# A fused attention and expert kernel: positions ahead of scaling, and transposes of zeros in the opening's idle stretches of the matmul engine

## The chip, the cores and the metric

The kernel runs on one core of a Trainium2 chip. The metric is the device time of one execution in microseconds (us); for the kernel before it is the median of three runs. The profile is of one execution, and its times count from the start of that execution's span. Engines are named TensorE (PE, with PEld for its weight loads), VectorE (DVE), ScalarE (ACT), GpSimd (POOL) and SyncE (SP).

## The reference

Three stages follow one another. The first is a linear attention with a complex decay for each position and dimension, the second a choice of one expert out of eight per token, the third a feed forward layer.

```python
mag = np.sqrt(a_re * a_re + a_im * a_im)
scale = np.minimum(mag, 0.999) / (mag + 1e-06)
for t in range(S):                      # B, H, S, D = 4, 8, 768, 48
    S_re = ar * S_re - ai * S_im + k[t] v[t]^T
    S_im = ar * S_im + ai * S_re
    y[t] = q[t] @ S_re
x = y as (3072, 384)
e = argmax(x @ w_gate);  x = gate_w * sigmoid(x @ w_output_gate) * relu(x @ w1[e]) @ w2[e]
out = max(0.01 * (x @ w_in), x @ w_in) @ w_out
```

## The kernel before

The kernel does not run the recurrence step by step. It takes chunks of 128 positions, 24 in all (`NCH`), where chunk `n` belongs to batch `n % 4`. Within a chunk the logarithm of the decay and its angle are summed over positions by a matmul with the triangle `tri`. Queries are multiplied by the exponential of the summed logarithm (`fall`), keys by its inverse (`rise`); that is `scale` (L883). Both are rotated by the summed angle (`rotate`, L896). Then the chunk is an ordinary masked attention plus a state carried from chunk to chunk.

The coefficients `a_in` pass through a long chain of elementwise work, in units of one chunk (the first two) or two chunks: squares and logarithms on ScalarE (L636 to L646), the signed numerator, the cap and the negative logarithm on VectorE (`numerator` L841, `cap` L848, `decay_log` L855), a difference and a product on GpSimd (`cosine_log` L483, `sine_eps` L492), the tangent of half the angle on VectorE (L862), the arctangent on ScalarE (L656) and the turn on VectorE (L870). GpSimd's `sine_eps(u)` waits, from unit 3 on, for the count `s_qe` of scaled queries, that is for `scale(n + 1)` of the chunk in which it stands.

TensorE sums the logarithms (`sum_logs`, L1096) and the turns (`sum_turns`, L1106); each sum is one call, which the profile shows as two matmul records. It transposes rotated queries and keys (`transposes`, L1136 and L1138), which ScalarE and VectorE copy from the banks (`query` L696, `first_key` L703 into `k_t`, `second_key` L919), computes scores (L1119), outputs (L1164, L1169), the update of the state (L1178) and the logits (L1189, L1191). Each chunk is done in two halves of four heads.

Each engine works through an order written out by hand, and semaphores tie the orders together. The opening prepares units 0 to 2 and chunk 0 ahead of the loop; TensorE's part of it is seven calls (L1203 to L1209), each of which waits for its own input. In the loop VectorE's order for chunk `n` is: add the state's update, `mask`, `second_key`, the cap and the negative logarithm (even chunks), turns (odd chunks), `scale(n + 1)`, in some chunks `positions`, then `rotate(n + 1)` and the second mask.

`positions` (L946) belongs to the routing of tokens. For each group of four chunks TensorE computes ranks (`ranks`, L1200 and L1201), in chunks 6, 10, 14 and 18 ahead of the second scores, and VectorE makes positions of them with three instructions: a product, a sum, and a conversion to integers (L951). TensorE's update in that chunk waits for them (L1174), since the ranks lie in the same bank, and GpSimd needs them for the scatter of rows one chunk later. For the fifth group `positions` stands at L1035, ahead of the scaling, in chunk 21.

`zeros` is a tile of 128 x 386 which SyncE stores past the end of the sorted rows (L446) and, later, behind each expert's region. It is written in GpSimd's order behind the first six elementwise passes and the triangle `stri`.

Behind the attention come a table of blocks, the experts' two layers (L2060, L2070, L2082) with weights that GpSimd splits into two parts (L1843, L1845) into a buffer that TensorE has released, and the feed forward layer (L2102, L2115).

Of the kernel before, what the change touches and what calls it, by code (L numbers as in the profile page):

```python
# [17 lines left out]
C = P  # L18
# [164 lines left out]
def attention(nc, ctx, sem, sb, in_a, in_qkv, wg_pairs, bank, ident, tri, stri, ones, wgp_sb, flag, stage, wm, moe_w, xs,  # L183
# [3 lines left out]
    sc_bank, y_bank, u_bank, cum_bank = bank[4], bank[5], bank[6], bank[7]  # L187
# [65 lines left out]
    s_lnu = sem("log_of_square")  # L253
# [3 lines left out]
    s_nl = sem("neglog_ready")  # L257
    s_flip = sem("left_half_plane")
    s_num = sem("signed_imaginary_part")
# [58 lines left out]
    def fallen(n):  # L318

        if n == 0:  # L320
            return [2, 3, 4, 5]
        return [n + 4, n + 5] if n % 2 == 0 and n + 4 < NCH else []
# [142 lines left out]
    def scan_gpsimd(pool):  # L465
# [3 lines left out]
        pool.memset(log_eps[:, :], math.log(MAG_EPS)).then_inc(s_bias, 1)  # L469
        pool.memset(rounder[:, :], ROUND).then_inc(s_bias, 1)  # L470
        pool.memset(least_run[:, :], 3.0e38).then_inc(s_bias, 1)
        pool.memset(tri[:, :], 1.0).then_inc(s_const, 1)
        pool.memset(ident[:, :], 0.0).then_inc(s_const, 1)
        pool.wait_ge(s_const, 2)
# [91 lines left out]
        for u in range(3):  # L566
# [3 lines left out]
        pool.wait_ge(s_const, 6)  # L570
        pool.affine_select(out=stri[:, :], in_=stri[:, :], compare_op=ALU.is_gt, fill=0.0, base=0,
                           pattern=[[1, P]], channel_multiplier=-1).then_inc(s_const, 1)
        pool.memset(zeros[:, :], 0.0).then_inc(s_idle, 1)
        pool.iota(order[:, :], [[-1, E]], base=E, channel_multiplier=0,
                  allow_small_or_imprecise_dtypes=True).then_inc(s_k, 1)
        pool.iota(region[:, :], [[REG, E]], base=0, channel_multiplier=0,
# [242 lines left out]
    def scan_vector(dve):  # L819
# [63 lines left out]
        def scale(m):  # L883
            if not real(m):
                return
            dve.wait_ge(s_qkv[m % RING], 16 * (m // RING + 1))
            dve.wait_ge(s_rise, m + 1)
            need(dve, s_kr, 2 * m)
            dve.tensor_tensor(kh_bank[:, 0:W], qkv_in[m % RING][:, 1, :], rise[m % FALLS][:, :],
                              ALU.mult).then_inc(s_ke, 1)  # L890
            dve.wait_ge(s_fall, m + 1)
            need(dve, s_qr, 2 * m)
            dve.tensor_tensor(qh_bank[:, 0:W], qkv_in[m % RING][:, 0, :], fall[m % FALLS][:, :],
                              ALU.mult).then_inc(s_qe, 1)
# [51 lines left out]
        def positions(g):  # L946
            ranked = by_token(ranked_parts, g, E)
            dve.wait_ge(s_rank, g + 1)
            step(dve.tensor_tensor(ranked, ranks_at(g), of_group(pick, g), ALU.mult))
            step(dve.tensor_reduce(of_group(posf, g), ranked, AX_X, ALU.add))  # L950
            dve.tensor_copy(of_group(pos, g), of_group(posf, g)).then_inc(s_pos, 1)  # L951
# [74 lines left out]
        for n in range(NCH + 1):  # L1026
            add_update(n - 1)
            if n % 2 == 1:
                out_copy(n - 1)
            mask(n, 0)  # L1030
            second_key(n)
            if n % B == 3 and B < n < NCH - 1:
                gate_rows(n // B - 1)
            if n in (NCH - 3, NCH - 1):
                positions(GLAST - 2 + (n - NCH + 3) // 2)  # L1035
            if n == NCH - 2:
                gate_rows(GLAST - 2)
            if n == NCH:
                gate_rows(GLAST - 1)
                pick_experts(GLAST)  # L1040
                region_ends()
                positions(GLAST)
                gate_rows(GLAST)
            if chain_exp(n) is not None:
                cap(chain_exp(n))
                decay_log(chain_exp(n))
            if chain_angle(n) is not None:
                turns(chain_angle(n))
            scale(n + 1)
            if n % B == 2 and B < n < NCH - 2:  # L1050
                positions(n // B - 1)
            if n % 2 == 0:
                rotate(n + 1)
                mask(n, 1)
                u = chain_exp(n)
                if u is not None:
                    half_tangent(u)
                for m in summed(n):
                    phases(m)
                if n % B == 0 and 0 < n < NCH:  # L1060
                    pick_experts(n // B - 1)
                if n == NCH - 2:
                    pick_experts(GLAST - 1)
            else:
                rotate(n + 1)
                mask(n, 1)
                u = chain_log(n)
                if u is not None:
                    left_half(u)
                    sum_squares(u)  # L1070
                for m in summed(n):
                    phases(m)
                if u is not None:
                    numerator(u)
            if n in (NCH - 3, NCH - 2):
                first_trailing(n - NCH + 3)
            if n == NCH - 3:
                dve.wait_ge(s_u, len(units))
                dve.tensor_scalar(strong[:, :], least_run[:, (len(units) - 1) % 2:(len(units) - 1) % 2 + 1], WEAKEST,
                                  None, ALU.is_gt).then_inc(s_strong, 1)  # L1080
            if n == NCH - 2:

                dve.wait_ge(s_weak, 1)
                dve.tensor_scalar(flag[:, :], cum_bank[0:1, 0:1], float(P), None, ALU.is_lt).then_inc(s_flag, 1)

    def scan_tensor(pe):
        pe.wait_ge(s_const, 4)

        def sum_logs(m):
            pe.wait_ge(s_nl, unit_of(m) + 1)  # L1090
            if m == 3:
                pe.wait_ge(s_ph, 3)
            if m > 3:
                pe.wait_ge(s_kt[1], m - 3 - m % 2)
                pe.wait_ge(s_qt, 2 * (m - 3 - m % 2))
            pe.matmul(cum_of(m, 0)[:, 0:W], tri[:, :], neglog[pair(unit_of(m))][:, ccols(m)], start=True,  # L1096
                      stop=True).then_inc(s_cl, 1)

        def sum_turns(m):
            pe.wait_ge(s_turn, unit_of(m) + 1)  # L1100
            need(pe, s_carried, m - B + 1)
            if m in (2, 3):
                pe.wait_ge(s_rise, 1 if m == 2 else 4)
            if m > 3:
                pe.wait_ge(s_ph, m)
            pe.matmul(cum_of(m, 1)[:, 0:W], tri[:, :], turn[pair(unit_of(m))][:, ccols(m)], start=True,  # L1106
                      stop=True).then_inc(s_ct, 1)
# [15 lines left out]
        def transposes(n, h):  # L1123
            if not real(n):
                return
            pe.wait_ge(s_qr, 2 * (n + 1))
            pe.wait_ge(s_kr, 2 * (n + 1))
            need(pe, s_qt, 2 * n + h)
            if n == 0:
                pe.wait_ge(s_ph, 2)  # L1130
            need(pe, s_kt[1 - h], n + h)
            if h == 0 and n % 2 == 1 and n + 3 < NCH:
                pe.wait_ge(s_rise, n + 5)
            for a in range(HH):
                head = h * HH + a
                pe.transpose(qt_bank[0:2 * D, a * C:(a + 1) * C],  # L1136
                             qr[n % 2][:, head, :, :].rearrange("p c d -> p (c d)"), ident[:, :])
                last = pe.transpose(kt_bank[0:2 * D, a * C:(a + 1) * C],  # L1138
                                    kr[n % 2][:, head, :, :].rearrange("p c d -> p (c d)"), ident[:, :])
            last.then_inc(s_tqk, 1)  # L1140
# [54 lines left out]
        def ranks(g):  # L1195
# [4 lines left out]
            pe.matmul(ranks_at(g), stri[:, :], of_group(pick, g), start=True, stop=False)  # L1200
            pe.matmul(ranks_at(g), ones[:, :], acc[:, n * E:(n + size) * E], start=False, stop=True).then_inc(s_rank, 1)  # L1201

        sum_logs(0)  # L1203
        sum_logs(1)
        sum_turns(0)
        sum_turns(1)
        sum_logs(2)
        sum_turns(2)
        transposes(0, 0)  # L1209

        for n in range(NCH + 1):
            scores(n, 0)
            if n == 0:
                sum_logs(3)
            transposes(n, 1)
            logits(n - 1)
            if n % B == 2 and B < n < NCH - 2:
                pe.wait_ge(s_su, min(n, LAST))
                ranks(n // B - 1)
            if n in (NCH - 3, NCH - 1):  # L1220
                pe.wait_ge(s_su, LAST)
                ranks(GLAST - 2 + (n - NCH + 3) // 2)
            scores(n, 1)
            for m in fallen(n):
                if m > 3:
                    sum_logs(m)
            outputs(n, 0)
            if n % 2 == 0:
                for m in summed(n):
                    sum_turns(m)  # L1230
            transposes(n + 1, 0)
            if n % 2 == 1:
                for m in summed(n):
                    sum_turns(m)
            if n == NCH - 2:
                pe.wait_ge(s_strong, 1)
                pe.wait_ge(s_const, 7)
                pe.wait_ge(s_ph, NCH)
                pe.matmul(cum_bank[:, 0:1], ones[:, :], strong[:, :], start=True, stop=True).then_inc(s_weak, 1)
            outputs(n, 1)  # L1240
# [971 lines left out]
```

## Time and profile before

| | us |
|---|---|
| median of three runs | 1013.23 |
| lowest and highest | 1013.14, 1015.47 |
| the profiled execution, its own time | 1014.68 |
| its span, first to last instruction | 1012.7 |
| TensorE busy (matmuls) | 941.1, 93% |
| GpSimd, ScalarE, VectorE busy | 505.5, 453.9, 415.9 |

The span has four stretches. The opening lasts until the loop over chunks is under way, some 45 us. The attention runs to about 293 us. Some 20 us of table, tails and first block follow, in which TensorE has almost nothing to do, and then the experts and, from 593 us, the feed forward layer, with TensorE busy throughout. A busy TensorE in this profile is not TensorE at its peak: the same matmuls take twice as long at the lower of its two clocks.

A row of a timeline gives the start, the duration (of several instructions in a row, if they are merged: x4), the engine, the line, the operation and the tiles, and in brackets how long the engine had idled and what ended that. A row of the chain gives start, length and the piece of work that the end of the program waited for. Clock columns give the granted clock as a share of the full 2.4 GHz.

### The profile page before, as it was taken

How to read it: one execution, taken by the hardware profiler on the slowest of the kernel's cores; microseconds unless marked ns; L12 is line 12 of the kernel's file. 1: busy time of each engine (PE TensorE's matmuls, PEld its weight loads, DVE VectorE, ACT ScalarE, POOL GpSimd, SP SyncE). 2: the span in 40 equal slices, each digit the busy share in tenths (PEclk: the TensorE clock that was granted, in tenths of full speed). 3: DMA queues.
4: the chain of work that ended last, by engine and by line, in shares of the span. 5: the costliest groups of instructions: out<-in, count | busy, mean ns of one | idle time of the engine just before them, and what ended most of it. 6: DMA issues, size and time to landing. Idle time of an engine off the chain costs nothing.

```text
span 1012.7 us, 17328 instructions
## 1 busy us (share of the span) xinstructions
PE 941.1 (93%) x5836; PEld 832.5 (82%) x5837; DVE 415.9 (41%) x742; ACT 453.9 (45%) x772; POOL 505.5 (50%) x429
## 2 busy tenths in 40 slices
PE   1899999999838999999999999999999999999995
PEld 0677778887736999998998989999999999999995
DVE  6698998998844233233232322212112121121110
ACT  7899888897612232232222333333333333333322
POOL 4134565565556568568839943342342433433433
PEclk9999999999978999999999999999999999999998
DMA  4542463430252343343534520010010100000000
GB/s 149 166 134 80 124 214 103 112 110 17 100 171 96 106 163 107 103 163 104 155 114 163 186 57 17 16 39 16 9 39 17 39 16 17 32 1 1 32 1 32
DMA packets 47190, 84.04 MB, mean 83 GB/s; under 512 B 23812, under 2 KB 36376, under 8 KB 44568
## 3 DMA queue, kind: packets, MB, share of 16 engines
q1 hardware_dynamic: 40984, 48.59, 16.0%
q0 software_dynamic: 6144, 34.65, 9.7%
q8 instruction: 37, 0.61, 0.3%
q14 instruction: 25, 0.20, 0.1%
HBM read 65.80 MB, written 17.38 MB: 82 GB/s over the span
## 4 chain that ended last, share of the span: by engine, by line
PE 72%; ACT 10%; issue 6%; DVE 6%; POOL 4%; SPq 1%; DMA 1%; POOLq 0%; DVEq 0%; ACTq 0%
PE bank L2102 20%; PE bank L2115 19%; PE bank L2060 11%; PE bank L2082 10%; POOL wm L1845 3%; PE bank L2070 2%; PE bank L1136 1%; PE bank L1119 1%; PE bank L1138 1%; POOL wm L1843 1%; PE bank L1096 1%; DVE neglog L848 1%; PE bank L1178 1%; PE bank L2036 1%; PE bank L1106 1%
## 5 line engine op out<-in xcount | busy, mean ns | idle before, releaser
L1871 POOL TENSOR_TENSOR act_r<-act_f,act_r 128x512 fp32r<-128x512 f32 x96 | 124.4, 1296 | 260.5 <-ACT act_r L1930 257.8
L2115 PE MATMUL bank<-w_out_r,act_r 128*128 128x384 f32 x1152 | 217.7, 337 | 0.3 <-POOL act_r L1871 0.3
L2102 PE MATMUL bank<-x,w_in_r 128*128 128x512 f32 x864 | 216.7, 395 | 0.0
L2115 PEld LDWEIGHTS bank<-w_out_r,act_r 128*128 128x128 f32 x1152 | 204.8, 188 | 8.8 <-POOL act_r L1871 0.6
L1991 DVE TENSOR_TENSOR act_f<-bank,small 128x512 f32<-128x512 f32 x96 | 66.4, 692 | 292.7 <-ACT small L1927 275.2
L2102 PEld LDWEIGHTS bank<-x,w_in_r 128*128 128x128 f32 x864 | 159.6, 188 | 29.4
L1927 ACT ACTIVATE small<-bank 128x512 f32<-128x512 f32 x96 | 57.4, 598 | 191.5 <-PE bank L2102 191.4
L2060 PE MATMUL bank<-wm,x_tr 128*128 (+1 forms) x522 | 129.1, 401 | 4.0 <-POOL wm L1845 1.7
L2082 PE MATMUL bank<-wm,h_tr 128*128 (+1 forms) x696 | 128.6, 339 | 0.7 <-DVE h_tr L1975 0.7
L2082 PEld LDWEIGHTS bank<-wm,h_tr 128*128 128x128 f32 x696 | 120.1, 188 | 1.0 <-issue 1.0
L2060 PEld LDWEIGHTS bank<-wm,x_tr 128*128 128x128 f32 x522 | 97.6, 191 | 24.8 <-issue 5.0
L1845 POOL TENSOR_TENSOR wm<-stage,wm 128x3072 fp32r<-128x3072 f32 x14 | 95.3, 6808 | 1.2
L1930 ACT ACTIVATE act_r<-act_f 128x512 fp32r<-128x512 f32 x96 | 60.7, 632 | 72.8 <-DVE act_f L1991 72.8
L1907 ACT ACTIVATE h_tr<-bank 128x512 fp32r<-128x512 f32 x58 | 31.6, 596 | 120.5 <-PE bank L2070 120.5
L1843 POOL TENSOR_SCALAR wm<-stage 128x3072 fp32r<-128x3072 f32 x14 | 38.9, 2780 | 71.3 <-PE bank L2082 56.3
L1902 ACT ACTIVATE h<-bank 128x512 f32<-128x512 f32 x58 | 31.5, 596 | 71.4 <-PE bank L2060 71.4
L1119 PE MATMUL bank<-q_t,k_t 96*128 96x128 f32 x384 | 56.2, 291 | 4.5 <-ACT q_t L696 2.7
L1981 DVE COPY y_b<-bank 128x384 f32<-128x384 f32 x29 | 16.2, 558 | 95.1 <-PE bank L2082 80.4
L1136 PE MATMUL bank<-ident,qr 128*96 128x128 f32 x192 | 46.8, 282 | 7.3 <-DVE qr L911 7.3
L1119 PEld LDWEIGHTS bank<-q_t,k_t 96*128 96x128 f32 x384 | 48.3, 197 | 6.1 <-ACT q_t L696 4.2
L1966 DVE CAST x_tr<-bank 128x384 fp32r<-128x384 f32 x30 | 16.7, 558 | 80.5 <-PE bank L2036 80.5
L1975 DVE TENSOR_TENSOR h_tr<-bank,h_tr 128x512 fp32r<-128x512 f32 x58 | 37.4, 686 | 21.3 <-ACT h_tr L1907 21.0
(193 smaller groups left out, 1378.1 us busy)
## 6 DMA issues: line engine op xcount, KB each, us to landing
stage<-moe_w POOLq DMA_DIRECT2D x12, 1536.0 KB, 7.0
qkv_in<-in_qkv SPq DMA_DIRECT2D x24, 576.0 KB, 5.5
a_in<-in_a SPq DMA_DIRECT2D x11, 768.0 KB, 5.3
stage<-moe_w SPq DMA_DIRECT2D x4, 1536.0 KB
x_b<-x_sorted SPq DMA_DIRECT2D x30, 193.0 KB
y_sorted<-y_b SPq DMA_DIRECT2D x29, 192.0 KB
xg<-y_sorted SPq DMA_DIRECT2D x24, 192.0 KB, 2.4
stage<-w_out POOLq DMA_DIRECT2D x2, 1536.0 KB, 7.1
```

The source lines that it names most:

```text
L1119: last = pe.matmul(sc_bank[:, a * C:(a + 1) * C], k_t[h][:, a * C:(a + 1) * C], q_t[h][:, a * C:(a + 1) * C], start=True, stop=True)
L1136: pe.transpose(qt_bank[0:2 * D, a * C:(a + 1) * C], qr[n % 2][:, head, :, :].rearrange("p c d -> p (c d)"), ident[:, :])
L1843: pool.tensor_scalar(lead, half, 1.0, 0.0, ALU.mult, ALU.add).then_inc(s_ws, 1)
L1845: pool.tensor_tensor(trail, half, lead.bitcast(F32), ALU.subtract).then_inc(s_wh, 1)
L1871: pool.tensor_tensor(a[:, 1, :], act_f[f % 2][:, :], a[:, 0, :].bitcast(F32), ALU.subtract).then_inc(s_gl, 1)
L1927: act.activation(small[f % 2][:, :], h_bank[f % 2][:, :], ACT.Copy, scale=0.01).then_inc(s_c, 1)
L1930: act.activation(act_r[f % 4][:, 0, :], act_f[f % 2][:, :], ACT.Copy).then_inc(s_gh, 1)
L1991: dve.tensor_tensor(act_f[f % 2][:, :], h_bank[f % 2][:, :], small[f % 2][:, :], ALU.max).then_inc(s_g, 1)
L2060: last = pe.matmul(hid_bank[j][:, :], x_tr[:, xp, t * P:(t + 1) * P], wmf[:, part_of(base, wp * WE + t * F1 + j * 512, 512)], start=(t == ...
L2082: last = pe.matmul(ye_bank[:, 0:W], h_tr[:, hp, t * P:(t + 1) * P], wmf[:, part_of(base, wp * WE + t * W, W)], start=(t == 0 and n == 0), ...
L2102: last = pe.matmul(h_bank[f % 2][:, :], w_in_r[:, wp, t * F2 + f * P:t * F2 + (f + 1) * P], window_part(w, xp)[:, t, :], start=(t == 0 and ...
L2115: last = pe.matmul(o_bank[j][:, 0:W], a[:, ap, j * P:(j + 1) * P], w_out_r[:, wp, f * W:(f + 1) * W], start=(f == 0 and n == 0), stop=(f = ...
```

## The change

`positions` goes ahead of `scale(n + 1)` in VectorE's order, in chunks 6, 10, 14 and 18. TensorE gets eleven groups of transposes, 144 in all, each behind a wait for a count that another engine raises. They read the tile of zeros and write into the output bank, which holds zeros until chunk 0's outputs. The memset of the zeros moves to the start of GpSimd's order, since the transposes read the tile from the first group on. In the loop only chunk 0 has groups of transposes.

```diff
@@ scan_gpsimd
         pool.memset(least_run[:, :], 3.0e38).then_inc(s_bias, 1)
+        pool.memset(zeros[:, :], 0.0).then_inc(s_idle, 1)
         pool.memset(tri[:, :], 1.0).then_inc(s_const, 1)
...
-        pool.memset(zeros[:, :], 0.0).then_inc(s_idle, 1)
@@ scan_vector
                 turns(chain_angle(n))
-            scale(n + 1)
             if n % B == 2 and B < n < NCH - 2:
                 positions(n // B - 1)
+            scale(n + 1)
@@ scan_tensor
+        def keep_warm(count, event, value):
+            pe.wait_ge(event, value)
+            for i in range(count):
+                pe.transpose(y_bank[:, i % 4 * C:(i % 4 + 1) * C], zeros[:, 0:C], ident[:, :])
+        pe.wait_ge(s_clear, 1)
+        pe.wait_ge(s_idle, 1)
+        keep_warm(28, s_num, 1)
         sum_logs(0)
         sum_logs(1)
+        keep_warm(20, s_nl, 2)
+        keep_warm(16, s_ratio, 1)
+        keep_warm(8, s_ratio, 2)
+        keep_warm(14, s_atan, 2)
         sum_turns(0)
         sum_turns(1)
         sum_logs(2)
+        keep_warm(8, s_rnd, 1)
+        keep_warm(10, s_rnd, 2)
         sum_turns(2)
+        keep_warm(10, s_turn, 3)
         transposes(0, 0)
+        keep_warm(16, s_qr, 2)
         for n in range(NCH + 1):
             scores(n, 0)
             if n == 0:
                 sum_logs(3)
             transposes(n, 1)
+            if n == 0:
+                keep_warm(8, s_qt, 1)
             logits(n - 1)
...
             scores(n, 1)
+            if n == 0:
+                keep_warm(6, s_lnu, 4)
             for m in fallen(n):
```

The counts are `s_num` of numerators, `s_nl` of negative logarithms, `s_ratio` of tangents, `s_atan` of arctangents, `s_rnd` of rounded angle sums, `s_turn` of turns, `s_qr` of rotated halves of queries, `s_qt` of copies into `q_t`, and `s_lnu` of logarithms.

## Rows read from the trace of the kernel before

**Rows 1.** The page: the chain by engine, and the weights' first pass on GpSimd.
```profile
PE 72%; ACT 10%; issue 6%; DVE 6%; POOL 4%; SPq 1%; DMA 1%; POOLq 0%; DVEq 0%; ACTq 0%
...
L1843 POOL TENSOR_SCALAR wm<-stage 128x3072 fp32r<-128x3072 f32 x14 | 38.9, 2780 | 71.3 <-PE bank L2082 56.3
```

**Rows 2.** The chain that ended last, 22 to 60 us: start, length, piece.
```profile
23.49 2.94 PE bank L1106 x4
...
30.87 0.45 PE bank L1136
...
32.85 0.60 ACT q_t L696
...
34.03 2.05 PE bank L1119 x8
36.07 1.28 PE bank L1096 x2
...
41.93 2.00 PE bank L1096 x4
```

**Rows 3.** The timeline of the opening, rows of four engines.
```profile
7.20 1.02 DVE L841 SCALAR_TENSOR_TENSOR a_in<-flip,a_in 128x384 f32<-128x384 f32 x2
...
14.24 2.90 PE L1096 MATMUL bank<-neglog,tri 128*128 128x384 f32 x4 [14.24 <-DVE neglog L855]
...
20.65 0.94 ACT L656 ACTIVATE main<-main 128x384 f32<-128x384 f32 x2
...
21.20 0.41 POOL L573 MEMSET zeros<- 128x386 f32 x1
...
37.15 1.81 POOL L483 TENSOR_TENSOR main<-main,log_sq 128x768 f32<-128x768 f32 x1 [14.57 <-ACT main L642]
...
39.10 0.59 ACT L696 ACTIVATE q_t<-bank 96x512 f32<-96x512 f32 x1 [1.27 <-PE bank L1138]
...
40.28 0.96 DVE L855 SCALAR_TENSOR_TENSOR neglog<-neglog,eps_mag 128x768 f32<-128x768 f32 x1
```

**Rows 4.** Busy time, clock and DMA by stretch, around the attention's end.
```profile
289.00:290.00 1.00, 0.00 (x0) 0.00 (x0) 0.58 (x4) 0.40 (x3) 0.71 (x3) 0.50 0.28 105
...
313.00:314.00 1.00, 1.00 (x6) 0.84 (x5) 0.00 (x0) 0.00 (x0) 0.95 (x1) 1.00 0.00 0
```

**Rows 5.** Transposes of 128x128: timeline at the low clock, chain at full clock.
```profile
305.54 0.90 PE L2036 MATMUL bank<-ident,x_b 128*128 128x128 f32 x3 [13.10 <-ACT x_b L1897]
...
345.14 0.87 PE bank L2070 x8
```

**Rows 6.** The timeline of chunk 6, and of chunk 21's conversion.
```profile
101.33 1.82 POOL L483 TENSOR_TENSOR main<-main,log_sq 128x768 f32<-128x768 f32 x1
...
102.29 1.27 DVE L848 TENSOR_SCALAR neglog<-log_sq 128x768 f32<-128x768 f32 x1
...
104.61 1.56 PE L1096 MATMUL bank<-neglog,tri 128*128 128x384 f32 x4 [0.33 <-DVE neglog L855]
...
105.67 1.81 POOL L492 TENSOR_TENSOR a_in<-a_in,eps_mag 128x768 f32<-128x768 f32 x1 [2.53 <-DVE bank L893]
...
105.86 1.66 DVE L951 CAST pos<-posf 128x4 int32<-128x4 f32 x1
...
107.57 0.88 PE L1178 MATMUL bank<-qkv_in,kr 128*96 128x48 f32 x8 [0.38 <-DVE pos L951]
...
111.03 0.58 ACT L703 ACTIVATE k_t<-bank 96x512 f32<-96x512 f32 x1
...
264.56 0.17 DVE L951 CAST pos<-posf 128x4 int32<-128x4 f32 x1
```

**Rows 7.** The conversion's line over the whole span.
```profile
L951 DVE CAST pos<-posf x7: 169/1659/1668, 105.9 to 293.0; 128x4 int32<-128x4 f32 x5, 128x2 int32<-128x2 f32 x2
```

**Rows 8.** The chain of chunk 8.
```profile
126.95 1.56 PE bank L1096 x4
...
132.45 0.58 ACT k_t L703
```

## The prediction

> **What bounds the kernel now.** I read the page first. The chain that ended last is 72% TensorE, and where it passes through GpSimd, which splits the experts' weights, that work waited for TensorE to release a buffer [rows 1]. So behind the attention nothing runs on a clock of its own, and a shift made early should arrive at the end. The change works before 44 us and at four points of the attention; the question is what the chain goes through there.
>
> The chain of the opening [rows 2] goes through TensorE in five pieces between 23.49 and 43.93 us, with short pieces of ScalarE and VectorE between them, and TensorE's pieces are slow. Four records of the turn sums take 2.94 us; four of the same shape take 1.56 in chunk 8 [rows 8]: a factor of 1.88. The clock column of the opening is no help (it shows 1.00 before the first matmul has run); where it does report, it falls from 1.00 to 0.50, the 1.2 GHz level, when the attention's matmuls stop, and is back at 1.00, 2.4 GHz, at 313 us, after work that began at 305.54, with one pause [rows 4, 5]. The opening's durations are those of the low level. The last piece holds the return: four records in 2.00 us are two at 0.64, as at 36.07, and two at 0.36, so the clock rose near 43.2. Before that TensorE idled until 14.24, and again from 17.14, where the log sums end, to 23.49, 6.35 us [rows 2, 3].
>
> Chunk 6 shows the other part [rows 6, 7]. VectorE's conversion of positions, 128x4 elements, takes 1.66 us. Of seven the median is 1659 ns and the shortest 169, so four are long. The long one starts at 105.86, behind the start of GpSimd's product (105.67), and ends at 107.52 with it (107.48). That product waits for `scale(n + 1)`, and `positions` stands right behind `scale(n + 1)`: they meet each time. It reaches the chain: from the start of the log sums to the copy into `k_t` chunk 6 takes 111.03 - 104.61 = 6.42 us, chunk 8, which has no positions, 132.45 - 126.95 = 5.50 [rows 8].
>
> **Positions ahead of scaling.** Nothing is added; three VectorE instructions pass two others, in chunks 6, 10, 14 and 18. They wait for the ranks, which stand in TensorE's queue ahead of a set of scores of about 1 us that is done 0.33 before 104.61; VectorE arrives at 104.5. No wait is added. GpSimd is idle for the 2.53 us before its product, so the conversion finds it idle. From the conversion to the next instruction is 1.57 us today (to 107.43, where the product releases it) and 0.11 behind a short one (chunk 21, where it stands ahead of the scaling) [rows 6]. VectorE gains 1.46. The scaling comes about 0.56 later: the conversion's 0.11 and two small steps of some 0.22. Three things hang on it: GpSimd's product (from 106.2 to 108.0, and the pass that needs it comes near 108.4), ScalarE's fall of chunk `n + 5` (behind log sums that end at 106.17, the scaling ends at 106.0), and the rotation, done near 107.9. Each has room. TensorE gains less than VectorE: its stall of 0.38 before the update goes, and then it is itself what is late, with update and turn sums in front of the next transposes. That is chunk 8's pattern, so I take the difference of the two chunks, 0.92. Bounds: 0, if the conversion stays long against something else, and 1.46, all that VectorE gains. 4 x 0.92 = 3.7 us, between 0 and 5.8.
>
> **The memset moved.** 0.41 us on GpSimd [rows 3], now ahead of `tri` and `ident`, which are ready some 2 us into the span and first wanted at 7.7; the bias columns, for which ScalarE waits, are written before it. Where it stood, GpSimd idles for 14.57 us afterwards. Nothing either way.
>
> **144 transposes.** A 128x128 transpose costs 0.21 at the low clock (three take 0.90 with the tail of the last, about 0.47) and 0.109 at the full one (eight take 0.87) [rows 5]. The first 28 follow the first numerator, at 7.7 us, and take 6.0 at the low clock, to 13.7, in front of the log sums at 14.24. From 7.7 on TensorE is all but never idle. The clock came back 7.5 us after the start of such work at 305.54, so I expect it by 15 to 17. Then come 20 (2.2 us), 16 (1.7), 8 (0.9), and 14 (1.5) behind the second arctangent at 21.6 [rows 3], done by 23.2: the turn sums lose nothing. From there, in order.
>
> Turn sums: 2.94 becomes 1.56, 1.4 gained, and phases, turns and the rotation follow, ended by 29.45. TensorE meanwhile does a log sum (25.05 to 25.8), 8 and 10 transposes (27.7), a turn sum (28.5) and 10 more: 29.6, so 0.15 is lost. The eight transposes of chunk 0, 1.96 today, take 1.0 and end at 30.6 instead of 32.83: 2.2 earlier.
>
> ScalarE's two copies would let the scores start at 31.8, but 16 transposes last until 32.35: 1.7 earlier. Scores, a log sum and eight transposes, 5.04 today (34.03 to 39.07), take 2.65 and end at 35.0: 4.1 earlier.
>
> Now ScalarE is late. It ends its exponential 1.27 before the copy at 39.10 [rows 3], at 37.83, and follows its own `k_t` copy, so 35.6: the copy starts at 35.65, 3.45 earlier. VectorE caps the logarithm meanwhile, and should meet GpSimd's difference (1.81 long [rows 3], from 34.95), as in chunk 6, where the cap takes 1.27 beside it [rows 6]; it ends at 36.8, and the pass behind it (0.96) has the negative logarithm ready at 37.8 instead of 41.24. Scores end near 37.45, six transposes at 38.1, and the log sums run to 39.7 instead of 43.93: 4.2 earlier. From here the work is the same, at the full clock.
>
> So 4.2 us. Upper bound: all slow pieces at the full clock and nothing lost, (2.94 + 1.96 + 5.04 + 2.05) x 0.47 + 0.44 = 6.1. Lower: 1.4, if the turn sums gain and groups that overrun eat the rest. Loads are no limit: each idle stretch in these rows ends with an engine.
>
> **Sum.** 4.2 + 3.7 = 7.9 us off the profiled execution's 1014.68 (span 1012.7) is 1006.8. That execution is 1.45 above the median of the three, 1013.23, so the median comes to 1005.3.
>
> **A rule against it.** All that fills the gaps is transposes, and no stretch of the trace has transposes alone, so it cannot show that they raise the clock. From 34.03 to 39.07 TensorE was busy for 5.04 us, the last 1.7 transposes, and the clock was not up [rows 2]; real matmuls from 39.9 on brought it by 43.2. That suits transposes that don't count, and as well the pause before 39.9 that broke the stretch. The Trainium skill ("TensorE: Matmul & The Clock Gate", Part 4, PE-mode transpose) says that the full clock does not engage for transpose-mode work, as it does not count as busy in the same way. By that rule the kernel becomes slower, by the sum faster. The first rival is that mechanism, priced from rows.
>
> **Rivals.** *The clock stays low under the fillers* (slower). Its place is TensorE's queue from 17.1 on, where the log sums end at the low clock. 20 + 16 + 8 + 14 = 58 transposes of 0.213 last 12.4 us, to 29.5: the turn sums start 6.0 late. With 18 more, a turn sum and 10 more, chunk 0's transposes start at 40.6 instead of 30.87, 9.7 late. The 16 last 3.4 in a gap of 1.2 (11.9), the 8 last 1.7 in one of 0.8 (12.8), the 6 add 1.3: 14.1 late. Less 3.7 from the positions it is +10.4: 1023.6. It decides at the 14 behind the second arctangent: with the clock up by about 20 us they end in time; if it is down there, each group adds. For it: that stretch up to 39.07, and that the two returns seen come under real matmuls. Against it: a transpose is a matmul record on the same engine, and its time halves with the clock like theirs. 18%.
>
> *Only one part pays.* If the conversions stay long, 4.2 is left: 1009.0. If the fillers overrun and the opening gives only its lower bound, 1.4 + 3.7: 1008.1. For it: three groups lie within 0.5 us of their gap. 17%.
>
> *The gain is given back* (no change): TensorE goes to the low clock again after the attention [rows 4] and could come back later than at 313; most of the 7.9 would have to go there, and the time at the low clock is under 8 us of work. 7%.
>
> **How the numbers follow.** The sum's case has 58%, the partial ones 17%, no change 7%, the slow one 18%. The forecast is the sum's, 1005.3. Its own range is 1001.5 to 1008: the bounds 6.1 and 5.8 together would give 1001.3, 2 and 3 of the two parts 1008. With the partial cases the range is 1001.5 to 1010.2, and what it leaves out is the slow case and little else. A measurement of this kernel can tell about 0.3%, 3 us, from no change: faster, below 1010.2, 0.75; within 0.07; slower 0.18.
>
> **What would show it.** Right: the turn sums start by 23.6 and take about 1.56; the log sums end near 39.7; all conversions take 0.17, and chunk 6 has 5.5 us from log sums to `k_t`; the attention ends 7 to 9 us earlier and the stretch behind it is as long as before. Wrong: fillers at 0.21 us each and turn sums near 29 us; a conversion that still ends with a GpSimd operation; or a wait behind the attention that grew by what was gained.

## The result, and the profile after

| | before | after |
|---|---|---|
| median of nine runs each, us | 1014.38 | 1009.97 |
| lowest and highest | 1013.14, 1020.23 | 1007.20, 1013.18 |
| ratio, 95% interval | | 0.9939 (0.9915 to 0.9964) |
| the profiled execution's span | 1012.7 | 1005.5 |

The kernel is faster by 0.61%, 6.2 us by the ratio, with an interval from 3.7 to 8.6; the two medians differ by less, 4.4 us. The spans of the two profiled executions differ by 7.2 us. The nine times of the changed kernel lie up to 6 us apart, which the experiments come back to.

The opening, in TensorE's timeline of the changed kernel (start, duration, line, tiles, count; L1207 are the new transposes):

```profile
7.95 5.37 PE L1207 MATMUL bank<-ident,zeros 128*128 128x128 f32 x28 [7.95 <-DVE a_in L841]
...
14.20 1.56 PE L1096 MATMUL bank<-neglog,tri 128*128 128x384 f32 x4 [0.88 <-DVE neglog L855]
...
15.59 2.35 PE L1207 MATMUL bank<-ident,zeros 128*128 128x128 f32 x20
...
18.68 4.77 PE L1207 MATMUL bank<-ident,zeros 128*128 128x128 f32 x38 [0.73 <-DVE main L862]
...
23.58 1.56 PE L1106 MATMUL bank<-turn,tri 128*128 128x384 f32 x4
...
32.25 1.06 PE L1119 MATMUL bank<-q_t,k_t 96*128 96x128 f32 x8
...
38.64 1.56 PE L1096 MATMUL bank<-neglog,tri 128*128 128x384 f32 x4 [0.60 <-DVE neglog L855]
```

The first 28 transposes take 5.37 us, not 6.0. What happened inside shows when they are counted by stretch (busy time of PE and PEld with counts, clock, DMA):

```profile
8.00:11.00 3.00, 3.00 (x15) 3.00 (x16) 1.00 0.86 351
11.00:12.00 1.00, 1.00 (x6) 1.00 (x5) 1.00 0.10 41
12.00:13.00 1.00, 1.00 (x10) 1.00 (x9) 1.00 0.00 0
```

Five start in each microsecond at first (15 in three), then ten in one: the clock doubled near 12.3 us. TensorE had then done nothing since the start of the span but transposes of zeros. The clock column shows 1.00 on either side, as it did in the opening of before, so the rate of the records has to tell. (The counts of a stretch take in a record that began before it.) The log sums at 14.20 already take 1.56 us, as do the turn sums at 23.58, where [rows 2] had 2.94; those start 0.09 later than in [rows 2]. The log sums that started at 41.93 in the chain there end at 40.20 now, against 43.93.

The stretch where I had ScalarE late, and VectorE's cap beside GpSimd's difference (timelines of VectorE, ScalarE and GpSimd in the changed kernel):

```profile
35.48 2.12 DVE L848 TENSOR_SCALAR neglog<-log_sq 128x768 f32<-128x768 f32 x1
...
37.63 0.96 DVE L855 SCALAR_TENSOR_TENSOR neglog<-neglog,eps_mag 128x768 f32<-128x768 f32 x1
...
35.60 0.57 ACT L696 ACTIVATE q_t<-bank 96x512 f32<-96x512 f32 x1
...
35.01 2.16 POOL L484 TENSOR_TENSOR main<-main,log_sq 128x768 f32<-128x768 f32 x1 [12.70 <-ACT main L642]
```

The cap takes 2.12 us and ends at 37.60, 0.43 behind the difference, where I had let it end together with a difference of 1.81 us. The difference itself takes 2.16 us here. In chunk 6 of before it took 1.82 with a cap beside it [rows 6], so the cap alone does not explain the longer difference; its cause stays open.

In chunk 6 the rows are the ones that [rows 6 and 7] had, in the new order (VectorE, GpSimd, TensorE, ScalarE, and the conversion's line over the span):

```profile
101.21 0.17 DVE L951 CAST pos<-posf 128x4 int32<-128x4 f32 x1
...
102.52 1.83 POOL L493 TENSOR_TENSOR a_in<-a_in,eps_mag 128x768 f32<-128x768 f32 x1 [3.08 <-DVE bank L893]
...
100.91 1.56 PE L1096 MATMUL bank<-neglog,tri 128*128 128x384 f32 x4 [0.35 <-DVE neglog L855]
...
103.41 0.88 PE L1178 MATMUL bank<-qkv_in,kr 128*96 128x48 f32 x8
...
106.41 0.58 ACT L703 ACTIVATE k_t<-bank 96x512 f32<-96x512 f32 x1
...
L951 DVE CAST pos<-posf x7: 169/171/172, 101.2 to 285.6; 128x4 int32<-128x4 f32 x5, 128x2 int32<-128x2 f32 x2
```

The conversion is short in all seven places, TensorE's update at 103.41 has no wait in front, and from log sums to `k_t` it is 106.41 - 100.91 = 5.50 us, where [rows 6] gave 6.42. VectorE's rank steps come first, then the scaling, and GpSimd's product starts at 102.52, 1.14 us after the conversion has ended.

Behind the attention nothing changed in kind. The first block's transposes start at 298.16 instead of 305.54 [rows 5], 7.38 earlier, behind an idle stretch of 13.07 instead of 13.10 us. The span ends 7.2 earlier.

### The profile page after: what moved, and what is told of

It reads as the page before. It is cut to its first block, busy times and chain, and to the rows that moved or that the text cites. A ratio compares the mean times of both kernels' runs of the same rounds, so it can differ in the third digit from the quotient of the medians.

```text
span 1005.5 us, 17617 instructions
## 1 busy us (share of the span) xinstructions
PE 949.6 (94%) x5980; PEld 845.8 (84%) x5981; DVE 413.0 (41%) x742; ACT 454.2 (45%) x772; POOL 509.5 (51%) x429
## 4 chain that ended last, share of the span: by engine, by line
PE 74%; ACT 9%; DVE 5%; issue 5%; POOL 5%; SPq 1%; DMA 1%; POOLq 0%; DVEq 0%; ACTq 0%
PE bank L2123 20%; PE bank L2136 20%; PE bank L2081 11%; PE bank L2103 10%; POOL wm L1866 3%; PE bank L2091 2%; PE bank L1096 2%; DVE neglog L848 1%; PE bank L1178 1%; PE bank L1136 1%; POOL wm L1864 1%; PE bank L1164 1%; PE bank L1138 1%; PE bank L1106 1%; PE bank L1119 1%
```

## The experiments

To compare kernels whose input lands at slightly different moments, I read differences inside one execution: **the opening** from the first log sums (14.24 in before) to those of chunk 2 (62.77), the **attention** from there to the log sums of chunk 18 (234.83), and **the rest** from there to the end of the span. All are starts of rows of `sum_logs` in the timelines (L1096; L1102 in two of the kernels). Each row of the table is one execution.

| profiled execution | opening | attention | rest | span |
|---|---|---|---|---|
| before | 48.53 | 172.06 | 777.9 | 1012.7 |
| before, again | 46.84 | 172.11 | 778.0 | 1011.0 |
| changed | 44.85 | 169.35 | 777.1 | 1005.5 |
| changed, again | 44.84 | 169.37 | 778.8 | 1007.1 |
| transposes only | 44.86 | 172.13 | 776.8 | 1008.1 |
| positions only | 46.87 | 169.29 | 778.1 | 1008.6 |
| two steps ahead, conversion behind | 47.47 | 168.85 | 778.9 | 1009.6 |
| conversion inside the rotation | 44.85 | 171.56 | 781.7 | 1012.4 |
| only the first 28 | 47.51 | 169.32 | 777.1 | 1008.4 |
| without the first 28 | 45.97 | 169.35 | 777.0 | 1006.6 |
| without the 16 | 44.56 | 169.33 | 776.9 | 1006.4 |
| clock held at the end | 44.83 | 169.27 | 774.9 | 1003.8 |
| held, with both later edits | 44.56 | 169.33 | 774.8 | 1002.9 |

**The change again, and its halves.** Four kernels on one chip, with 17 runs of before (median 1013.44). The changed kernel:

> The changed kernel again, beside its two halves on one chip. If the shares add up and the rest of the spread is the clock's return behind the attention: the log sums of chunk 18 start 6.4 us earlier than before (at 228.4 in the span) in every execution, and the time is 5 to 7.5 us below the kernel before in executions whose return behind the attention takes equally long. If part of the gain is unstable in the opening: a clock rise later than 13 us in the opening's transposes and log sums of chunk 18 later than 228.6.

Six runs, 1006.01 to 1009.49, median 1008.25, 5.2 us below that of before; ratio 0.9938 (0.9926 to 0.9950), which is 6.3 us. The opening and the attention agree with the first profile to 0.02 us; the log sums of chunk 18 start at 228.27. So both gains repeat, and what differs between these two executions, 1.7 us, lies behind chunk 18. There the clock fell once in the attention's last chunks and again behind them (stretches; busy, clock):

```profile
277.00:279.00 2.00, 2.00 (x18) 0.50 0.94 358
...
283.00:285.00 2.00, 0.00 (x0) 0.57 0.01 3
...
306.00:307.00 1.00, 1.00 (x4) 0.50 0.00 0
...
307.50:309.00 1.50, 1.50 (x9) 1.00 0.00 0
```

**Only the transposes.**

```diff
+            scale(n + 1)
             if n % B == 2 and B < n < NCH - 2:
                 positions(n // B - 1)
-            scale(n + 1)
```

> Only the transposes and the memset; positions stay behind the scaling. Theory of two independent gains: the log sums that end at 43.93 end at 40.2, 3.7 earlier, and this shift arrives at the attention's end unchanged (3.5 to 3.9 us below before, ratio 0.9963). The four conversions stay at 1.66 us. Rival, the opening's gain is the whole of the change and positions only moves a wait: 6 to 7 us below before here.

Ratio 0.9987 (0.9975 to 1.0000), median 1011.45 of twelve runs: a gain of 1.3 us with an interval from none to 2.5 (the medians differ by 2.0), less than I had expected. The profile shows the shift as expected: opening 44.86, log sums at 38.74, the attention as in before. The conversions are long again, 1661 ns in the median. The times reach from 1010.30 to 1016.93, and the two highest belong to the executions with the lowest mean clock (0.980 and 0.978, where the others have 0.983 to 0.987). So part of the shortfall stands in executions that spent more time at the low clock. Where in the span they spent it, no profile of them shows; every profiled execution with all eleven groups has its low stretches behind 276 us and none in the opening. The other part is that I had measured the gain from one opening of before.

**Only positions.**

```diff
             if n % B == 2 and B < n < NCH - 2:
                 positions(n // B - 1)
+            scale(n + 1)
             if n % 2 == 0:
```

> Only positions ahead of scaling; no transposes. Theory: 0.91 us in each of four chunks, so 3.6 us by the attention's end (ratio 0.9964), the four conversions at 0.17 us, and nothing earlier than chunk 6; the opening as before, the last log sums of the opening ending at 43.9. Rival, the gain needs the opening's shift: 0 to 1 us.

Ratio 0.9965 (0.9951 to 0.9978), 3.5 us, six runs. The attention takes 169.29, 2.8 less for the three chunks it spans, 0.92 each. That settles this half. The opening, though, took 46.87 us and not 48.53, with no edit in it, which I had not expected.

**The kernel before, again.**

> The kernel before once more, for the clock of its unfilled opening. Theory: without transposes the moment of the rise varies between executions (38.4, 39.1, 39.6 and 43.2 us in the four unfilled openings seen), so the time from the first log sums to those of chunk 2 lies anywhere from 46.8 to 48.6 us, while filled openings have 44.85. Rival, the kernel before has 48.5 whatever the execution, and the shorter openings belong to the edits of the others.

46.84 us: the theory holds, and the other openings without the later groups had 46.87, 47.47 and 47.51. The stretches of its opening (busy, clock), and a row of its turn sums:

```profile
28.00:31.00 3.00, 1.17 (x4) 1.00 0.27 7
31.50:38.00 6.50, 5.29 (x21) 0.50 0.94 288
38.50:41.00 2.50, 1.59 (x10) 1.00 0.96 357
```

```profile
26.07 1.49 PE L1096 MATMUL bank<-neglog,tri 128*128 128x384 f32 x2
...
28.41 0.91 PE L1106 MATMUL bank<-turn,tri 128*128 128x384 f32 x2 [0.85 <-DVE turn L870]
```

The 1.00 of the first stretch says nothing by itself, since the column reads 1.00 until its first change. The durations do: two records of log sums at 26.07 still take 1.49 us, two of the turn sums at 28.41 take 0.91, where the other execution of before had 1.65. So here the clock rose at about 28 us, fell again near 31.4 and rose for good at 38.3, five microseconds sooner than in the execution that the prediction read. An unfilled opening is left to the moment at which the clock happens to rise; the filled one takes 44.83 to 44.86 in five executions with all eleven groups. The transposes therefore gain 2.0 to 3.7 us, by which execution of before one compares with, and 3.7 is the most of the five seen (counting the kernel with two steps ahead and the one with only the first 28, both below).

**Is it the collision?** Two kernels ask why the conversion was long. In the first, on the kernel before, only the two small steps go ahead:

```diff
+            if n % B == 2 and B < n < NCH - 2:
+                positions(n // B - 1)      # product and sum
             scale(n + 1)
             if n % B == 2 and B < n < NCH - 2:
-                positions(n // B - 1)
+                convert(n // B - 1)        # conversion alone
```

> The kernel before, with the product and the sum of positions ahead of the scaling in chunks 6, 10, 14 and 18, and the conversion alone behind it. Theory, the conversion's length is a collision with GpSimd's product that starts as the scaling ends: the conversion starts beside the product and takes 1.6 to 2.0 us again, TensorE's update still waits for it, chunk 6 keeps 6.4 us or slightly more from log sums to k_t, and the span is within 1 us of before. Rival, the gain comes from doing the rank steps earlier whatever the conversion meets: 5.5 us in chunk 6 and 3 us or more off the attention.

It was not long, and the attention took 168.85 us, 0.4 to 0.5 less even than in the kernels with `positions` ahead of the scaling; that is one execution, and why was not asked. My expectation failed, but on its premise: behind the scaling the conversion starts at 104.90 and GpSimd's product at 105.16 (timelines of VectorE and GpSimd).

```profile
104.90 0.16 DVE L953 CAST pos<-posf 128x4 int32<-128x4 f32 x1
...
105.16 1.83 POOL L492 TENSOR_TENSOR a_in<-a_in,eps_mag 128x768 f32<-128x768 f32 x1 [2.97 <-DVE bank L893]
...
105.44 0.55 DVE L906 TENSOR_TENSOR qr<-bank,sin 128x384 f32<-128x384 f32 x1
```

Without the two steps in between it slips in ahead of the product. The last row shows what the collision is not: an instruction of the rotation, which reads a bank and one tile, takes 0.55 us in the middle of the same product, as the other three of the rotation do. So not every VectorE instruction beside it is held up. Both theories are still alive, and a second kernel puts the conversion inside the product for certain:

```diff
         dve.tensor_tensor(kr[n % 2][:, :, 1, :], ...).then_inc(s_kr, 1)
+        if then is not None:
+            convert(then)
```

> The changed kernel with the conversion alone moved into the rotation, behind its first instruction, some 0.5 us behind the scaling's end and so inside GpSimd's product, which starts 0.26 us behind it; the two small steps stay ahead of the scaling. Theory, the collision with that product is what made the conversion long and the chunk slow: it takes about 1.5 us in four chunks and ends with the product, chunk 6 takes 6.3 to 6.5 us from log sums to k_t, and from the log sums of chunk 2 to those of chunk 18 it is 172 us instead of 169.35. Rival, the order of the rank steps is the cause: the conversion at 0.17 us, or long with chunk 6 still at 5.5 us.

```profile
102.69 1.64 DVE L955 CAST pos<-posf 128x4 int32<-128x4 f32 x1
...
102.48 1.82 POOL L493 TENSOR_TENSOR a_in<-a_in,eps_mag 128x768 f32<-128x768 f32 x1 [2.97 <-DVE bank L893]
...
100.97 1.56 PE L1102 MATMUL bank<-neglog,tri 128*128 128x384 f32 x4 [0.34 <-DVE neglog L855]
...
107.38 0.58 ACT L703 ACTIVATE k_t<-bank 96x512 f32<-96x512 f32 x1
```

The conversion takes 1.64 us and ends at 104.33, the product at 104.30. Chunk 6 takes 107.38 - 100.97 = 6.41 us from log sums to `k_t`, and the attention 171.56, 2.2 longer than in the changed kernel (172 was expected). The rank steps stand ahead of the scaling here as in the changed kernel. So the cause is the overlap with GpSimd's product, not the place of the rank steps.

**How many transposes does it need?** Only the first group, the other ten taken out:

> The changed kernel with only the first group of 28 transposes; the ten later groups are left out. Theory, the later groups keep the clock up through pauses such as 15.8 to 23.5 us: the clock rises near 12 us and falls again before the turn sums, which take 2.9 us; the opening's gain shrinks from 3.7 to 0.5 to 1.5 us. Rival, one rise is enough for the whole opening: the turn sums take 1.56 us and the gain stays at 3.7 or grows.

The first log sums take 1.56 us, the turn sums 2.93, behind 7.78 us of idleness, and the opening is 47.51, no better than unfilled ones:

```profile
8.20 5.01 PE L1207 MATMUL bank<-ident,zeros 128*128 128x128 f32 x28 [8.20 <-DVE a_in L841]
...
14.44 1.56 PE L1096 MATMUL bank<-neglog,tri 128*128 128x384 f32 x4 [1.24 <-DVE neglog L855]
...
23.78 2.93 PE L1106 MATMUL bank<-turn,tri 128*128 128x384 f32 x4 [7.78 <-DVE turn L870]
```

The later groups are what keeps the clock. Without the first group, the others kept:

> The changed kernel without the first group of 28. Theory: the first log sums take 2.9 us at the low clock, the 20 transposes behind them run at 0.21 us, the clock rises by 20 us and the turn sums are at the full clock; the groups in front of them end near 23.5 to 24.5, so 0 to 1 us of the opening's 3.7 is lost. Rival of the prediction, the clock stays down under transposes that start late: turn sums near 27 to 29 us and the opening slower than before.

```profile
14.34 2.90 PE L1096 MATMUL bank<-neglog,tri 128*128 128x384 f32 x4 [14.34 <-DVE neglog L855]
...
17.03 8.05 PE L1207 MATMUL bank<-ident,zeros 128*128 128x128 f32 x58
...
24.92 1.46 PE L1106 MATMUL bank<-turn,tri 128*128 128x384 f32 x4
```

The log sums take 2.90, the clock rises near 20 us under the transposes, the turn sums start at 24.92 and take 1.46, and the opening is 45.97: 1.1 us lost, mostly groups that started at the low clock and overran. It is a little more than expected, and far from the rival. Without the 16:

```diff
         transposes(0, 0)
-        keep_warm(16, s_qr, 2)
```

> The changed kernel without the group of 16 between the first transposes and the first scores, which overran its gap by 0.5 us. Theory, VectorE's cap waits there for GpSimd's difference and hides the overrun: the scores start 0.5 us earlier and the opening's last log sums start at 38.6 as in the changed kernel, within 0.2. Rival, the overrun is on the chain: they start at 38.1, and the span is 0.5 us shorter. If the clock falls in the pause of 1.2 us instead, the scores take 2 us.

```profile
33.25 1.13 PE L1119 MATMUL bank<-q_t,k_t 96*128 96x128 f32 x8 [1.22 <-ACT q_t L696]
```

The opening is 44.56, 0.3 shorter: between the two expectations, and the clock did not fall in the pause of 1.22 us in front of the scores. The overrun is on the chain in part.

**Holding the clock behind the attention.** The times of the changed kernel spread, and its clock is low from 282 to 306 us. So 132 more transposes there, into the bank of the scores:

```diff
+        hold_clock(20)
         pe.wait_ge(s_acc, GLAST + 1)
...
         ranks(GLAST)
+        hold_clock(112)
```

> The changed kernel and 132 more transposes of zeros, into the score bank: 20 in the pause before the token counts and 112 behind the last ranks, some 12.2 us in a gap of 13.1. Theory, the spread and a further loss come from the clock that is low from 282 to 306 us: the clock stays at 1.00 there, the first 18 matmuls of the experts take 4.4 us instead of 6.9, eight transposes 0.87 instead of 1.15, the span is 3 to 3.5 us below the changed kernel's 1005.5, and the times spread by 1 us or less. Rival, spread and gap come from the transfers between (store of the tails, load of the first block), which the clock does not touch: no more than 1 us below the changed kernel and the same spread.

Median 1006.51 of five runs, 1005.80 to 1007.77; ratio to before 0.9931 (0.9918 to 0.9944). The rest shrinks by 2.3 us against the changed kernel's first profile (777.1) and by 4.0 against its second (778.8); that is less, for the first, than the 3 to 3.5 expected, because the clock stayed up only until the first block:

```profile
282.00:296.00 14.00, 13.94 (x128) 1.00 0.50 170
...
300.50:303.00 2.50, 2.50 (x7) 0.50 0.18 64
...
299.65 5.96 PE L2087 MATMUL bank<-wm,x_tr 128*128 128x512 f32 x18 [1.33 <-DVE x_tr L1995]
```

The low stretch begins behind a pause of 1.33 us in front of the first layer. The last kernel fills that too, and leaves the 16 out:

```diff
         transpose_block(0)
+        for i in range(12):
+            pe.transpose(ye_bank[:, i % 4 * P:(i % 4 + 1) * P], zeros[:, 0:P], ident[:, :])
         layer1(0)
```

> The changed kernel without the group of 16, with the 132 transposes at the attention's end of the run before, and 12 more between the first block's transposes and its first layer, a pause of 1.33 us in which the clock fell once more at 300 us. Theory: the clock stays at 1.00 from the opening's rise to the end, the first 18 matmuls of the experts take 4.4 us instead of 6.0, the opening is 0.3 us shorter; the time is 3.5 to 5 us below the changed kernel's, near 1004.5, and the times spread by about 1 us. Rival, the rest of the spread comes from transfers: the clock is at 1.00 and the times still spread by 2 us.

```profile
297.97 1.47 PE L2167 MATMUL bank<-ident,zeros 128*128 128x128 f32 x12
...
299.47 4.36 PE L2086 MATMUL bank<-wm,x_tr 128*128 128x512 f32 x18
...
307.45 4.37 PE L2086 MATMUL bank<-wm,x_tr 128*128 x18 [1.36 <-DVE x_tr L1994]
```

In this execution the clock is at 1.00 until TensorE's work is over, and the first 18 matmuls take 4.36 us, as expected. But the rest is 774.8, against 774.9. The second block's layer now waits 1.36 us for VectorE. VectorE has worked on the table of blocks until 304.60 and begins the two passes that the layer needs only at 306.09, without a wait that the profile names; the kernel before this one has the same pause of 1.5 us there. So what TensorE saved it waits for.

Median 1006.89, ratio 0.9931 (0.9917 to 0.9946), times from 1005.41 to 1008.56. The expectation of 1004.5 and of a spread of 1 us was wrong. Only the profiled execution is known to have kept its clock. It is the fastest of the five and has a mean clock of 0.996, while the two slowest, 1008.50 and 1008.56, have 0.993 and 0.992. So in those the clock was low for longer, and where is not shown. The two kernels with a held clock are the fastest of those run more than once, but their intervals overlap that of the changed kernel, so that they beat it is likely and not shown.

**What the rests have in common.** The table's last stretch orders itself by how long the granted clock stood at 0.50 between 270 and 315 us:

| low for about, us | kernels | rest, us |
|---|---|---|
| 0 | held, with both later edits | 774.8 |
| 3 | clock held at the end | 774.9 |
| 20 | transposes only | 776.8 |
| 24 | before twice, changed, positions only, and the three that leave groups out | 776.9 to 778.1 |
| 27 | changed again; two steps ahead | 778.8, 778.9 |
| 34 | conversion inside the rotation | 781.7 |

Part of the differences is the fourth conversion, in chunk 18: it is long in both executions of before, in transposes only and in the last row, and costs some 0.9 us there, if it costs what the other three do. The order follows the clock.

## Why the prediction was right, and where not

The direction and both mechanisms held; the size was too large. The forecast took 7.9 us off one execution, and the two profiled ones differ by 7.2, but that agreement is partly luck, since the execution of before had the longest opening of all (see the baseline below). The measured 1009.97 is 4.7 us above the predicted 1005.3 and lies 0.2 us inside the end of the range, 1010.2; three of the nine runs lie beyond it. Of the 4.7 us, 1.5 to 2.2 are gain that was not there: 7.9 against 5.7 to 6.4, as worked out below. The remaining 2.5 to 3.2 stand in neither part of the change, by these figures. The forecast rested on a median of before from three runs, and that of nine is 1.15 higher; and the changed kernel's own times reach over 6 us, longer as their mean clock is lower.

**Positions.** 0.92 us a chunk was predicted from chunk 8's pattern; [rows 6 and 8] against the changed chunk 6 give 6.42 - 5.50 = 0.92, and the half alone 3.5 us. The rule to take TensorE's gain, not VectorE's 1.46, was what made this right. The collision was read correctly from one coinciding end and four long durations, and the kernel with the conversion inside the rotation bears it out.

**Fillers cost nothing at the turn sums.** Held: 23.58 against 23.49. The clock was expected by 15 to 17 and rose at 12.3. The memset at the head of GpSimd's order shows nowhere: the log sums start at 14.20, against 14.24.

**The rule against it.** The first rival, that transposes do not bring the clock up, is refuted here: by the trace of the changed kernel it rose under 4.4 us of nothing but transposes of zeros. The Trainium skill ("TensorE: Matmul & The Clock Gate", Part 4, PE-mode transpose) says otherwise; the measurement decides, for the transposes of fp32 in this kernel. The trace calls them MATMUL, as it does every matmul, so whether they run in the mode that the page means is not shown. The rival's 18% was not far too much for what the trace of before could show, but its point of decision was never near: even without the first group the turn sums started at 24.92, not 29.5.

**The opening's 4.2 us.** It came out as 3.7 in that pair of executions. The mis-sized term is the cap: I let it end with GpSimd's difference at 36.8, and it ended at 37.6, so that the last log sums started at 38.64 and not at 38.1. Half of the 0.8 us was a misreading: in [rows 6] the cap ends at 103.56 and the difference at 103.15, so a cap that meets the difference ends 0.41 behind it, not with it. The other half is the difference, 2.16 us long where 1.81 was taken. The copy into `q_t` started at 35.60, predicted 35.65; the scores at 32.25, predicted 32.35. The 0.5 us charged to the 16 transposes was 0.3 on the chain.

**The baseline.** This is the larger error. The step "4.2 + 3.7 = 7.9 off the profiled execution" took the opening of one execution, 48.53 us, as the kernel's own. Of the five openings without the later groups it is the longest; the others are 46.84 to 47.51. I had seen that the rise of the clock inside the opening is an event, and not asked whether it comes at the same moment each time. Against the other four the transposes are worth 2.0 to 2.7 us, and with 3.7 for positions 5.7 to 6.4. The ratios of both series lie there (6.2 and 6.3 us); their medians differ by less (4.4 and 5.2 us). The halves alone sum to 4.8 us by their ratios and 5.2 by their medians, but each ratio is known to 1.3 us only.

**After the attention** the shift arrived whole, as argued from the wait of the weights for TensorE. The third rival, a later return of the clock there, does happen, but from execution to execution rather than because of the change: the low stretch lasts 24 us in both executions of before, 24 and 27 in the changed kernel. The mean clocks of the changed kernel's nine runs go from 0.985 at 1007.2 us down to 0.978 at 1013.2. In the kernel before the mean clock does not order the times so (1014.02 us at 0.985, 1012.90 at 0.980). Its openings blur the figure: in the first profiled execution the column reads 1.00 although the durations up to 43.2 us are those of the low clock, and in the second it shows a low stretch because the clock had risen and fallen again.

## What to carry to other kernels

Fill idle stretches of TensorE only where its matmuls are on the chain and run at half rate, and keep filling: one group raised the clock, and without the others it fell again before it was of use. Where two engines' instructions end together again and again, move the shorter one out of the other's way, even by half a microsecond, and expect the gain of the engine that is late next, not that of the one relieved. Before sizing such a gain, look whether the event it rests on comes at the same time in more than one execution. And where one engine's pass starts beside another's, read from a row where such a pair ends, not only that it meets.

## What the runs showed of the hardware

The clock of TensorE rose under fp32 transposes alone (at 12.3 us, begun at 7.95). In unfilled openings its moment differed by up to 15 us between executions of the same code (first rise near 28 us in one and 43.2 in another), and it fell back in between. A pause of 1.33 us in front of matmuls was followed by a low stretch in the held kernel; pauses of 1.22 us in the kernel without the 16 and of 1.36 us in the last kernel were not, so the length of the pause alone did not decide. Behind the attention the clock stood at its low level for 20 to 34 us in the profiled executions that do not fill the gap.

VectorE's conversion of 128x4 elements takes 0.17 us alone and 1.64 inside a 1.82 us product of GpSimd, and is short when it starts 0.26 us ahead of the product. The rotation's instructions, 128x384 from a bank and a tile, take 0.55 us inside the same product. The cap, 128x768 from one tile, takes 0.55 us alone and 1.27 or 2.12 beside GpSimd's difference, behind whose end it ends by 0.4 us each time; the difference took 2.16 us once, in the opening, and 1.82 in chunk 6.
